# Table buffers four deep, frequency rows read back three slots at a time

## What is computed

```
X  = rfft(x, axis=1)
Yr = Xr @ w_r - Xi @ w_i + b_r
Yi = Xr @ w_i + Xi @ w_r + b_i
Y  = sign(Y) * max(|Y| - 0.01, 0)          (both parts)
y  = irfft(Y, n=3008)
h  = y @ moe_w_in;   y1 = (h * cos(h)) @ moe_w_out
h2 = y1 @ moe2_w_in; y2 = (h2 * clip(h2 + 3, 0, 6) / 6) @ moe2_w_out
```

## Time and profile before

| | us |
|---|---|
| median of 3 runs | 1237.89 (1236.77 to 1238.49) |
| the profiled execution's own time | 1237.29 |
| its span | 1235.5 |
| TensorE busy | 1208.6 (98%) |
| ScalarE, VectorE, POOL busy | 625.5, 609.1, 562.0 |
| first slot's table rounded / last one's | 37.1 / 155.0 |
| sines begin | 170.7 |

### The profile page before, as it was taken

How to read it: one execution, slowest core, us unless ns; L and a number is a source line. 1 busy time by engine, 2 the same in 40 slices (tenths; PEclk the granted TensorE clock), 3 DMA queues, 4 the chain that set the end, 5 groups by cost and what they waited for, 6 DMA issues and landing times.

```text
span 1235.5 us, 14644 instructions
## 1 busy us (share of the span) xinstructions
PE 1208.6 (98%) x5576; PEld 1007.8 (82%) x5576; DVE 609.1 (49%) x596; ACT 625.5 (51%) x703; POOL 562.0 (45%) x294
## 2 busy tenths in 40 slices
PE   8999969999999999999999999999999999999998
PEld 8866759888888888888888888888888888888886
DVE  2767826755444435445445355344354354454344
ACT  2655645665554445455445455455554454555443
POOL 2566745766444444444444444444444444444410
PEclk9999979999999999999999999999999999999999
DMA  9376525000000100100100001001001001000000
GB/s 260 117 207 195 178 39 205 18 1 1 30 1 1 35 1 0 34 0 0 34 0 20 14 0 34 0 0 34 0 0 34 0 0 34 0 1 18 1 18 18
DMA packets 28836, 48.79 MB, mean 39 GB/s; under 512 B 3327, under 2 KB 10111, under 8 KB 28800
## 3 DMA queue, kind: packets, MB, share of 16 engines
q1 hardware_dynamic: 28620, 48.06, 13.0%
q10 hardware_dynamic: 180, 0.25, 0.2%
HBM read 30.21 MB, written 17.43 MB: 39 GB/s over the span
## 4 chain that ended last, share of the span: by engine, by line
PE 91%; DMA 3%; DVE 2%; ACT 2%; SPq 1%; issue 1%; POOL 0%; DVEq 0%; ACTq 0%
PE banks L582 41%; PE banks L633 40%; DMA dbs<-in_db 3%; PE banks L560 2%; PE banks L487 2%; PE banks L502 1%; PE banks L503 1%; PE banks L507 1%; PE banks L522 1%; PE banks L523 1%; DMA v<-y 1%; PE banks L472 1%; ACT abh L711 0%; DVE phase L960 0%; DVE ga L978 0%
## 5 line engine op out<-in xcount | busy, mean ns | idle before, releaser
L1120 POOL TENSOR_TENSOR gal<-ga,gah 128x1024 fp32r<-128x1024 f32 (+1 forms) x93 | 222.2, 2390 | 514.1 <-ACT gah L801 514.1
L956 DVE SCALAR_TENSOR_TENSOR phase<-phase,banks 128x1024 f32<-128x1024 int32 (+1 forms) x96 | 114.9, 1197 | 273.3 <-ACT phase L785 273.3
L1126 POOL TENSOR_TENSOR gbl<-gb,gbh 128x1024 fp32r<-128x1024 f32 (+1 forms) x88 | 208.0, 2363 | 16.6 <-ACT gbh L835 16.6
L793 ACT ACTIVATE cosine<-phase,half_pi 128x1024 f32<-128x1024 f32 (+1 forms) x96 | 109.1, 1136 | 193.2 <-DVE phase L960 192.5
L785 ACT ACTIVATE phase<-banks 128x1024 int32<-128x1024 f32 (+1 forms) x96 | 97.0, 1011 | 155.5 <-PE banks L582 154.8
L978 DVE TENSOR_TENSOR ga<-banks,cosine 128x1024 f32<-128x1024 f32 (+1 forms) x96 | 115.4, 1202 | 104.9 <-ACT cosine L793 97.2
L1019 DVE SCALAR_TENSOR_TENSOR gb<-ramp,banks 128x1024 f32<-128x1024 f32 (+1 forms) x96 | 115.1, 1199 | 103.5 <-ACT ramp L825 103.4
L825 ACT ACTIVATE ramp<-banks,three 128x1024 f32<-128x1024 f32 (+1 forms) x96 | 105.5, 1099 | 110.7 <-PE banks L582 110.7
L835 ACT ACTIVATE gbh<-gb 128x1024 fp32r<-128x1024 f32 (+1 forms) x96 | 99.9, 1041 | 36.7 <-DVE gb L1019 32.6
L582 PE MATMUL banks<-xl,w1h 128*128 128x512 f32 (+1 forms) x384 | 116.6, 385 | 0.0
L582 PE MATMUL banks<-xh,w_lo 128*128 128x512 f32 (+1 forms) x384 | 116.6, 385 | 0.0
(11 more groups left out here) (96 smaller groups left out, 1850.3 us busy)
## 6 DMA issues: line engine op xcount, KB each, us to landing
w<-in_w_ff SPq DMA_DIRECT2D x32, 256.0 KB, 6.3
xb<-in_x SPq DMA_DIRECT2D x32, 192.0 KB, 5.4
xf<-x_spill SPq DMA_DIRECT2D x11, 512.0 KB, 4.4
out_y<-yt SPq DMA_DIRECT2D x11, 512.0 KB, 3.4
y_spill<-y SPq DMA_DIRECT2D x21, 256.0 KB, 3.9
x_spill<-xs SPq DMA_DIRECT2D x11, 470.0 KB, 3.3
v<-y_spill SPq DMA_DIRECT2D x21, 240.0 KB
dbs<-in_db SPq DMA_DIRECT2D x24, 128.0 KB, 5.3
```

Source lines behind the costliest of these rows:

```text
L793: act.activation(cosine[:, :, 0:w], phase[:, :, 0:w], ACT.Sin, bias=half_pi[:, :], scale=-1.0).then_inc(a_cos, 1)
L956: dve.scalar_tensor_tensor(out=phase[:, :, 0:w], in0=phase[:, :, 0:w].bitcast(i32), scalar=-2.0 * math.pi, in1=bank[:, at:at + 2, 0:w], op ...
L1120: pool.tensor_tensor(gal[p % 2][:, :, 0:w], ga[:, :, 0:w], gah[p % 2][:, :, 0:w].bitcast(fp32), ALU.subtract).then_inc(a_gl, 1)
L1126: pool.tensor_tensor(gbl[pb % 2][:, :, 0:w], gb[:, :, 0:w], gbh[pb % 2][:, :, 0:w].bitcast(fp32), ALU.subtract).then_inc(b_gl, 1)
```

## The change

- `dbs` has `DBUF` = 4 buffers instead of two, placed over two chunks of the rounded weights that are filled only after the last slot. `load_db(i)` waits for `dft2(i - 4)` instead of `dft2(i - 2)`; four tables are loaded ahead of the loop.
- The order of the values is changed on the host (`im`), so that in `y_spill` the 24 full blocks of one r lie one behind the other. A row of `v` is 48 KB in one piece on both sides. The partition is now `5 * slot + r`: a slot's five are adjacent, and those of three slots are 15 in a row.
- `y_spill` has 130 rows a slot, so that the left blocks have five parts of two too; the two extra rows are filled once with numbers of the table (`pad_in`).
- Slots 0 to 20 are read back in seven batches of three, each with one full and one left read (720 KB and 60 KB instead of three times 240 and 16).
- Slots 21 and 22 are written and read back too: first their sine halves, each by itself, then both cosine halves in one read. Slot 23's cosine half is written and read last. `lay_full`, `lay_left` and the filler are gone; the sines contract over 115 rows.
- ACT issues no transfer; `copy_v(22)` stands ahead of `ab_high(23)`. POOL does `ys_low(22)` before one piece of the weights.

```
-        dbs_raw, dbs = zip(*[twice(f, f"dbs{i}", [P, 2, P]) for i in range(2)])
+        tables = Region(w1_at + (NWCH - 2) * WCH * 4)
+        dbs_raw, dbs = zip(*[twice(tables, f"dbs{i}", [P, 2, P]) for i in range(DBUF)])
...
             def load_db(i):
-                if i >= 2:
-                    sp.wait_ge(dft2_done, i - 1)
-                sp.dma_start(dbs_raw[i % 2][:, :, :], db[i, :, :, :]).then_inc(db_in[i % 2], 16)
+                if i >= DBUF:
+                    sp.wait_ge(dft2_done, i - DBUF + 1)
+                sp.dma_start(dbs_raw[i % DBUF][:, :, :], db[i, :, :, :]).then_inc(db_in[i % DBUF], 16)
...
-            def read_full(slot, i, first, count, done):
-                sp.dma_start(v[slot:slot + (GROUP - 1) * K1 + 1:K1, first:first + count, :],
-                             y_spill[i, GROUP * first:GROUP * (first + count), :].rearrange("(g r) n -> r g n", r=GROUP)
-                             ).then_inc(done, 16)
+            def read_full(slot, count, first, blocks, done):
+                at = y_spill[slot:slot + count, 0:GROUP * 2 * FULL, :].rearrange("s (r b) n -> s r b n", r=GROUP)
+                sp.dma_start(v[GROUP * slot:GROUP * (slot + count), first:first + blocks, :],
+                             at[:, :, first:first + blocks, :]).then_inc(done, 16)
...
+            def written(i):
                 sp.wait_ge(v_out[i % 2], 16 * (i // 2 + 1))
...
+            sp.dma_start(y_spill[:, P:ROWS, :], db[:, 0:4, :, :]).then_inc(pad_in, 16)
+            for i in range(DBUF):
                 load_db(i)
...
+            for i in range(LAST_K - 1):
+                if i + DBUF < K1:
+                    load_db(i + DBUF)
                 if i >= 1:
                     write_v(i - 1)
                 if i >= 2:
-                    read_v(i - 2)
+                    written(i - 2)
+                    if (i - 1) % BATCHED == 0:
+                        read_full(i - 1 - BATCHED, BATCHED, 0, 2 * FULL, v_in)
+                        read_left(i - 1 - BATCHED, BATCHED, 0, 2, v_in)
                     if i - 2 < NWCH:
                         load_w2(i - 2)
                 if i + 4 < NWCH:
                     load_w1(i + 4)
...
+            for i in range(LAST_K - 2, LAST_K):
+                write_v(i)
+            for i in range(LAST_K - 2, LAST_K):
+                written(i)
+                read_full(i, 1, FULL, FULL, v_sin_in)
+                read_left(i, 1, 1, 1, v_sin_in)
+            read_full(LAST_K - 2, 2, 0, FULL, v_cos_in)
+            read_left(LAST_K - 2, 2, 0, 1, v_cos_in)
+            write_v(LAST_K)
+            written(LAST_K)
+            read_full(LAST_K, 1, 0, FULL, v_cos_in)
+            read_left(LAST_K, 1, 0, 1, v_cos_in)
...
-            for par in range(2):
-                pe.wait_ge(v_in[par], 2 * 16 * len(range(par, LAST_K - 2, 2)))
-            pe.wait_ge(v_idle_in, 2 * 16)
-            for i in range(2):
-                pe.wait_ge(v_direct_in[i], (GROUP + 2) * 16)
+            pe.wait_ge(v_in, 2 * 16 * (LAST_K - 2) // BATCHED)
+            pe.wait_ge(v_sin_in, 2 * 2 * 16)
...
-            pe.wait_ge(v_last_in, (GROUP + 1) * 16)
+            pe.wait_ge(v_cos_in, 2 * 2 * 16)
...
-    order = [half * N2 + n for half in range(2) for n in range(GROUP * FULL)]
-    order += [half * N2 + n for half in range(2) for n in range(GROUP * FULL, N2)]
+    order = [half * N2 + GROUP * g + r for r in range(GROUP) for half in range(2) for g in range(FULL)]
+    order += [half * N2 + GROUP * FULL + r for r in range(LEFT) for half in range(2)]
```

More of the change, by code:

```diff
@@ L50 @@
 SBUF_S, SBUF_C, SBUF_X = 8, 2, 4
+DBUF, BATCHED = 4, 3
+ROWS = P + 2
 LAST_K = K1 - 1
@@ L70, in mixer_program @@
     x_spill = nc.dram_tensor("x_spill", [P, DC, TOKENS], fp32, kind="Internal").ap()
-    y_spill = nc.dram_tensor("y_spill", [K1, P, BATCH * DIM], fp32, kind="Internal").ap()
+    y_spill = nc.dram_tensor("y_spill", [K1, ROWS, BATCH * DIM], fp32, kind="Internal").ap()
     ctx = ExitStack()
@@ L192, in mixer_program @@
         v_out = [sem("v_out0"), sem("v_out1")]
-        v_in, v_last_in, v_idle_in = [sem("v_in0"), sem("v_in1")], sem("v_last_in"), sem("v_idle_in")
-        v_direct_in = [sem("v_direct_in0"), sem("v_direct_in1")]
-        db_in = [sem("db_in0"), sem("db_in1")]
+        v_in, v_sin_in, v_cos_in, pad_in = sem("v_in"), sem("v_sin_in"), sem("v_cos_in"), sem("pad_in")
+        db_in = [sem(f"db_in{i}") for i in range(DBUF)]
         w1_in, w2_in = [sem(f"w1_in{j}") for j in range(NWCH)], sem("w2_in")
@@ L241, in w2_chunks @@
             return tuple(range(first, min(first + (1 if G < PAIRS else 2), NWCH)))
[L244 to L252, removed]
         def x_slot(g):
@@ L368, in write_v, with read_left @@
                 sp.wait_ge(v_ready, i + 1)
-                sp.dma_start(y_spill[i, :, :], y[:, i, :]).then_inc(v_out[i % 2], 16)
-            def read_full(slot, i, first, count, done):
-                sp.dma_start(v[slot:slot + (GROUP - 1) * K1 + 1:K1, first:first + count, :],
-                             y_spill[i, GROUP * first:GROUP * (first + count), :].rearrange("(g r) n -> r g n", r=GROUP)
-                             ).then_inc(done, 16)
[L376 to L382, removed]
-                sp.wait_ge(v_out[i % 2], 16 * (i // 2 + 1))
[L384 to L388, removed]
-            for i in range(2):
+                sp.dma_start(y_spill[i, 0:P, :], y[:, i, :]).then_inc(v_out[i % 2], 16)
+            def read_full(slot, count, first, blocks, done):
+                at = y_spill[slot:slot + count, 0:GROUP * 2 * FULL, :].rearrange("s (r b) n -> s r b n", r=GROUP)
+                sp.dma_start(v[GROUP * slot:GROUP * (slot + count), first:first + blocks, :],
+                             at[:, :, first:first + blocks, :]).then_inc(done, 16)
+            def read_left(slot, count, first, blocks, done):
+                at = y_spill[slot:slot + count, GROUP * 2 * FULL:ROWS, :].rearrange("s (r b) n -> s r b n", r=GROUP)
+                sp.dma_start(v[GROUP * slot:GROUP * (slot + count), 2 * FULL + first:2 * FULL + first + blocks, :],
+                             at[:, :, first:first + blocks, :]).then_inc(done, 16)
+            def written(i):
+                sp.wait_ge(v_out[i % 2], 16 * (i // 2 + 1))
+            sp.dma_start(y_spill[:, P:ROWS, :], db[:, 0:4, :, :]).then_inc(pad_in, 16)
+            for i in range(DBUF):
                 load_db(i)
@@ L395, in _ @@
                 sp.dma_start(c2s[i][:, :], c2[i, :, :]).then_inc(c2_in, 16)
-            for i in range(K1 - 2):
-                load_db(i + 2)
+            sp.wait_ge(pad_in, 16)
+            for i in range(LAST_K - 1):
+                if i + DBUF < K1:
+                    load_db(i + DBUF)
                 if i >= 1:
@@ L405, in _ @@
                     load_w1(i + 4)
[L406 to L418, removed]
+            written(LAST_K - 3)
+            read_full(LAST_K - 2 - BATCHED, BATCHED, 0, 2 * FULL, v_in)
+            read_left(LAST_K - 2 - BATCHED, BATCHED, 0, 2, v_in)
+            for i in range(LAST_K - 2, LAST_K):
[10 more added lines that the diff above has]
+            read_left(LAST_K, 1, 0, 1, v_cos_in)
             def spill(g):
@@ L522, in dft2 @@
                     pe.matmul(o, das[:, const, :], part[par][:, 0, :], start=(n == 0), stop=False)
-                    mm = pe.matmul(o, dbs[par][:, const, :], part[par][:, 1, :], start=False, stop=(n == 2))
+                    mm = pe.matmul(o, dbs[i % DBUF][:, const, :], part[par][:, 1, :], start=False, stop=(n == 2))
                 mm.then_inc(dft2_done, 1)
@@ L556, in half_idft1 @@
             def half_idft1(g, at_bank, half, done):
-                k, n = part(g) * K1, part(g) * HALF
+                k, n = GROUP * (LAST_K if half else K1), part(g) * HALF
                 for j in range(BC):
@@ L713, in round_db @@
             def round_db(i):
-                act.wait_ge(db_in[i % 2], 16 * (i // 2 + 1))
-                act.activation(dbs[i % 2][:, :, :], dbs_raw[i % 2][:, :, :], ACT.Copy).then_inc(db_ready, 1)
+                act.wait_ge(db_in[i % DBUF], 16 * (i // DBUF + 1))
+                act.activation(dbs[i % DBUF][:, :, :], dbs_raw[i % DBUF][:, :, :], ACT.Copy).then_inc(db_ready, 1)
             def copy_v(i):
@@ L754, in _ @@
             copy_v(LAST_K - 2)
+            copy_v(LAST_K - 1)
             ab_high(LAST_K)
[L756 to L759, removed]
             weights_hi(LAST_K - 2)
@@ L1095, in _ @@
                 ys_low(i)
-                weights_lo(0, i - 1)
+            for i in range(LAST_K - 3, LAST_K - 1):
+                weights_lo(0, i)
             ys_low(LAST_K)
@@ L1155, in dft_constants @@
         to = slice(r * HALF, (r + 1) * HALF)
-        c2[0, r * K1:(r + 1) * K1, to] = weight * cos
-        c2[1, r * K1:(r + 1) * K1, to] = -weight * sin
+        c2[0, r:GROUP * K1:GROUP, to] = weight * cos
+        c2[1, r:GROUP * K1:GROUP, to] = -weight * sin
     cos, sin = turn(n2, k2, N2)
```

## The result

The changed kernel takes 1263.07 us (median of 4 runs, 1261.31 to 1263.75), the kernel before 1237.33 (1235.81 to 1238.49): a ratio of 1.0207, 95% interval 1.0189 to 1.0224. It is **slower by 25.7 us**. The forecast was 1252, in a range of 1229 to 1264. The profiled execution has a span of 1259.5 us, 24.0 more than before.

The account below looks back on a forecast made before the run. Five DMA engines, full throughout the row reads, were taken as the bound. Last read at 159 + 36.7 - 15.8 = 180, plus 5, starts sines at 185 (+14.3); 1237.3 + 14.3, and 0.6 for the median, gives 1252 us, range 1229 to 1264.

Parts of the forecast that it names:

- Three engines: Batched row reads: three engines carry each, the largest equal split fitting 3 source slots and 15 destination rows; today five.
- The price of a slot, 3.86 us: Row reads: a slot takes 3.86 us on three engines, 1.75 us more than today; 21 slots give +36.7 us.
- Stalls: Table waits: gone until about 90 us, then TensorE stalls 4 to 8 us every third step, once a batch.
- So the last batch lands at 180: End of row reads: today's last at about 159 us, plus 36.7, less 15.8, gives 180 us.
- five DMA engines are full for the whole stretch: Row-read stage today: v-row reads keep five of 16 DMA engines busy throughout, and the other eleven wait for them.
- the saving of 15.8 us: Batches: the others' transfers pass faster while thirteen engines idle; three quarters of a 21 us bound, -15.8 us.
- The last slots through DRAM, +5: End of stage: a write and two short reads take 5 us after the last batch, so sines start at 185.
- The cosines, 0, and 2 by the Trainium skill's port rule: Last cosine half: 0 us, ends -1 and +3; by the port rule slot 23's five adjacent rows cost 2 us more.
- the main case: Whole kernel: three engines, visibly slower, 1243 to 1262 us, likeliest 1252; chance 0.58.
- Three engines, but hidden: Rival: four buffers and lighter contention cover slower batches; sines at 171, 1236 to 1241 us; chance 0.08.
- Stalls that also cost clock: The long rival: stalls once a batch halve TensorE's clock, up to 3 us each over five; 1263 to 1275 us; chance 0.12.
- The faster rival: Batches spread over five engines or more, tables in time, table 23 rounded at 145.6; -9 to -11, 1227 us; chance 0.22.

Follow-up runs that it names:

- the cut reads: Each slot's read cut into rows 0 to 2 and 3 to 4, rows 24 apart: 1249.38 us with single-slot reads, 1269.65 us with three slots' reads issued together.
- The bunching kernel: Against the 1223.23 us kernel (four tables, slots read one by one into rows 24 apart), its reads issued three together every third step: 1234.34 us.

## Why the prediction was right, and where it was not

*Three engines.* Right: share 0.18 and 0.19, 69 and 72 GB/s, as forecast (0.19, some 70). The Trainium skill's rule of the common divisor ("DMA: Bandwidth & Descriptors", section "Why a DMA increments its semaphore by 16 and not by 1") holds for 5 (124 GB/s at 0.34), 3 and 15: going from three to fifteen took 27.8 us off, and going from five to three put 26 and 35 on. The same section lets a transfer use the lowest-numbered engines, and the cut reads agree: three pieces in flight.

*The price of a slot, 3.86 us.* High for a batch that is alone, fair for one among others. The packet records give 1.8 to 2.1 us for 63% of the 48 KB pieces (1.82 alone, 27 GB/s), and five at the median with their left blocks make 9.9 us a batch, 3.3 a slot. While other transfers pass a piece takes up to 3.4, and from the first piece's start to the last one's end the seven batches took 10.3 to 13.2 us, 3.4 to 4.4 a slot.

*Stalls.* Right in kind, place and size: good until 90 us, then 5.7 to 8.0 us once a batch.

*"So the last batch lands at 180".* This is the step that failed: it landed at 185.2. The sum stretched the old ring by its engine time and took batching as free ("I count it at nothing" was said of the issues, and nothing was set for the waiting). Two errors of opposite sign stood in it. The pace was better than forecast: the batches went out at 62.29 and 172.25 with five between, 18.3 us each or 6.1 a slot, where 3.86 + 3.5 - 0.75 gives 6.6. But a batch waits for its third slot, the first leaves at 62.29 where the kernel before sends its first read at 52.73, and the last is one lump of 13 us at the end with a write behind it. The bunching kernel prices that, for five engines and rows apart: 11.1 us. In the changed kernel it isn't priced by itself.

*The ground of the sum, "five DMA engines are full for the whole stretch".* The rows for it were read rightly, but they don't say that the engines set the pace. With four tables the same reads fit into 4.76 us. The 3.5 us a step for "the others" was thus not their need but included slack, and the saving of 15.8 us, three quarters of a gain on that slack, had no meaning of its own. A step's engine time is an upper bound while something else may hold it back.

*The last slots through DRAM, +5.* Measured 7.6, from the batch's landing at 185.2 to 192.76: 1.1 for the write, 6.5 for the reads. *The cosines, 0, and 2 by the Trainium skill's port rule.* Measured 1.9: the skill's figure was the better one. The last read lands in 5.34 us into neighbouring rows and in 3.0 us into rows apart (the kernel with slot 23's inverse step first). The sine read has the same penalty, 5.34 against 3.52 and 3.67. Together that is some 4 us that rows apart would save the changed kernel; with its own batches of three slots in one transfer this was not tried.

*Sum and rivals.* +22.0 and +1.9 instead of +14.3 and 0. The direction and the kind of loss came as forecast, the size 1.8 times as large. 1263 lies outside the main case's own range of 1243 to 1262; it is inside the stated one, by 0.9 us, because that took in a little of the long rival, and that much of it is luck. "Three engines, but hidden" is refuted. "Stalls that also cost clock" named 1263 to 1275 for the saving at a quarter or less, and 1263 is what came, but clock is a small part of it: the granted clock was 0.91 from 100 to 138 us and 0.93 from 138 to 164, so at most 3.4 + 1.8 = 5.2 of the 24.0 us went that way, and less where TensorE idled meanwhile. The faster rival needed more engines, and with them its mechanism came true: rounding of table 23 at 145.6 was forecast, 145.38 measured. That its time stayed at 1235 is put down to the bunching and the neighbouring rows at the end (the sines wait 12.9 us there); the two weren't taken apart in that kernel.

## What to carry to other kernels

Before merging transfers, count the engines that each side's outermost size allows, and look where the destination rows lie: the same bytes took 1223 us over five engines into rows apart, 1249 over three, and 1275 over five into neighbouring rows. A transfer on few engines is paid by every later one that spreads over all of them, so small and early beats large and late. When a stage shows a prefetch wait and a busy resource, deepen the prefetch by itself first: here that alone gave 9 us and told which of the two was the bound.

## What was not expected of the hardware

An issue can block. In the changed kernel SP's queue shows this, where seven transfers had just gone out behind a batch's two reads:

```profile
85.93 0.49 SPq L350 DMA_DIRECT2D dbs<-in_db  x1
86.46 7.51 SPq L360 DMA_DIRECT2D y_spill<-y  x1
```

The same issue takes 0.43 us at the median. It took 6.67 behind the next batch, again as the eighth transfer after it, and 7.35 and 6.45 at the same two places in the kernel that waits only ahead of a batch. Behind the third batch five transfers stood before it, and it took 0.51. The table issued at 83.98, in the same burst, took 15.32 us to land, and all that SP had to do stood behind the long issue. What it waits for isn't shown; it ended at 93.97, and from 91.9 us to then the packet records show nothing in flight but the batch's three pieces. And fifteen engines writing fifteen neighbouring rows were no faster than five writing rows apart: their 48 KB pieces took 6.0 us each in the mean, 15 x 49 kB / 6.0 = 123 GB/s, against 139 for the five in the row above. That kernel doesn't win by speed; its batches load fifteen engines alike, and no table comes late.
